# Own-place terms of two groups from scaled values, a one-step state update, and another order of work around the first bursts

## The reference

```python
for t in range(S):                      # attention with decay; state starts at 0
    y[:, :, t] = r_t . (state + (u * k_t) outer v_t)
    state = w * state + k_t outer v_t
x = y as 1536 rows of 384
p = probs / (sum(probs) + 1e-9)         # 4 experts
out = sum over e of p_e * (relu(x @ w1[e]) @ w2[e])     # 384 -> 1024 -> 384
h = out @ w_in;  result = (h * sigmoid(1.702 h)) @ w_out # 384 -> 2048 -> 384
```

## Time and profile before

| | us |
|---|---|
| median of 3 runs | 656.1 (653.75 to 657.89) |
| the profiled execution | 653.33 |
| its span, first to last instruction | 651.6 |
| PE busy in the span | 640.1 |
| DVE / ACT / POOL busy | 228.6 / 203.3 / 177.8 |
| mean granted clock of TensorE | 0.995 |

### The profile page before, as it was taken

The page is one execution under the profiler, slowest core; times in us unless marked ns, Lnnn a source line. Parts: engine busy times, 40 slices in busy tenths (PEclk is TensorE's granted clock), DMA queues, the critical chain, the costliest instruction groups (busy, mean ns, idle before and its releaser), DMA issues.

```text
span 651.6 us, 9471 instructions
## 1 busy us (share of the span) xinstructions
PE 640.1 (98%) x3886; PEld 540.4 (83%) x3887; DVE 228.6 (35%) x358; ACT 203.3 (31%) x429; POOL 177.8 (27%) x174
## 2 busy tenths in 40 slices
PE   7889999999999999999999999999999999999998
PEld 5789999988888888888888888888888888888886
DVE  8867666312122222222222222222543333333332
ACT  4544344232222211222211223222653333333332
POOL 6754320153234310434310436240770000000000
PEclk8999999999999999999999999999999999999999
DMA  8742343102300040100040000040000010001001
GB/s 312 297 154 86 128 175 133 52 2 94 149 1 1 12 184 0 49 0 1 9 185 1 0 1 1 11 185 0 1 0 1 1 48 1 1 1 48 1 1 48
DMA packets 8723, 38.69 MB, mean 59 GB/s; under 512 B 1504, under 2 KB 1632, under 8 KB 7392
## 3 DMA queue, kind: packets, MB, share of 16 engines
q1 hardware_dynamic: 8672, 38.00, 15.5%
HBM read 35.62 MB, written 2.38 MB: 58 GB/s over the span
## 4 chain that ended last, share of the span: by engine, by line
PE 95%; DVE 2%; issue 1%; ACT 1%; DMA 1%; SPq 0%; DVEq 0%; ACTq 0%
PE bank L1029 45%; PE bank L1053 30%; PE bank L1069 15%; PE bank L1099 2%; PE bank L1136 1%; PE bank L1139 1%; PE bank L1128 1%; ACT q_a_t L687 1%; DMA rk_in<-rk_t 1%; PE bank L1112 1%; DVE q_r_mid L760 0%; DVE q_a_t L842 0%; PE bank L1131 0%; DVE q_a_t L831 0%; DVE q_k_mid L757 0%
## 5 line engine op out<-in xcount | busy, mean ns | idle before, releaser
L1029 PE MATMUL bank<-x_hi,w_hi 128*128 128x512 f32 (+1 forms) x480 | 177.1, 369 | 0.2 <-DVE x_lo L779 0.2
L1029 PE MATMUL bank<-x_lo,w_hi 128*128 128x512 f32 (+1 forms) x480 | 177.0, 369 | 0.0
L1029 PE MATMUL bank<-x_hi,w_lo 128*128 128x512 f32 (+1 forms) x480 | 176.9, 369 | 0.0
L810 DVE SCALAR_TENSOR_TENSOR h_lo<-bank,h_hi 128x512 fp32r<-128x512 f32 (+1 forms) x112 | 68.8, 614 | 271.4 <-ACT h_hi L655 271.0
L655 ACT ACTIVATE h_hi<-bank 128x512 fp32r<-128x512 f32 (+1 forms) x112 | 59.9, 534 | 278.4 <-PE bank L1029 278.4
L579 POOL TENSOR_TENSOR w_lo<-staging,w_hi 128x384 fp32r<-128x384 f32 x80 | 82.2, 1039 | 167.5 <-ACT w_hi L625 167.5
L1053 PE MATMUL bank<-h_hi,w_hi 128*128 128x512 f32 (+1 forms) x336 | 121.9, 363 | 0.6 <-DVE h_lo L810 0.6
L1053 PE MATMUL bank<-h_lo,w_hi 128*128 128x512 f32 (+1 forms) x336 | 120.8, 360 | 0.0
L1053 PE MATMUL bank<-h_hi,w_lo 128*128 128x512 f32 (+1 forms) x336 | 120.8, 360 | 0.0
L1029 PEld LDWEIGHTS bank<-x_hi,w_hi 128*128 128x128 f32 x480 | 90.9, 189 | 15.3 <-issue 0.4
L1029 PEld LDWEIGHTS bank<-x_hi,w_lo 128*128 128x128 f32 x480 | 90.9, 189 | 14.9
(11 more groups left out here) (76 smaller groups left out, 447.5 us busy)
## 6 DMA issues: line engine op xcount, KB each, us to landing
staging<-weights SPq DMA_DIRECT2D x10, 1536.0 KB, 8.7
rk_in<-rk_t SPq DMA_DIRECT2D x12, 512.0 KB, 5.3
rkv_in<-rkv_n SPq DMA_DIRECT2D x10, 608.0 KB, 4.0
staging<-weights SPq DMA_DIRECT2D x4, 768.0 KB, 11.7
p_bc<-p_normalised SPq DMA_DIRECT2D x4, 768.0 KB, 4.4
out<-p_bc SPq DMA_DIRECT2D x9, 256.0 KB, 2.1
rkv_in<-rkv_n SPq DMA_DIRECT2D x2, 416.0 KB, 5.7
u_bc<-u_flat SPq DMA_DIRECT2D x1, 192.0 KB, 11.4
```

Of the source, the lines that this page charges most:

```text
L810: dve.scalar_tensor_tensor(h_lo[:, slot, 0:size], hid, 0.0, h_hi[:, slot, 0:size].bitcast(F32), ALU.max, ALU.subtract).then_inc(sem["hlo"], 1)
L1029: last = pe.matmul(bank[:, HID[j % 2], 0:tokens.stop - tokens.start], w[:, k, :], xs[c][:, k, tokens], start=(n == 0), stop=(n == 3 * KT - 1))
```

## The change

Groups 0 and 1 no longer have the own-place term in a_t. ACT zeroes `a_t[:, 0]` early, POOL zeroes `a_t[:, 1]`; DVE's `own_values` multiplies v by the result of first_diagonal, read from PSUM, into `v_first`, and PE adds it to the group's result with three 128x128 matmuls against the identity. ACT's `first_state` copies the first state. `carry` becomes four operations, one per pair of heads, new = old * w^128 + add; `fade` and `faded` go. The shares are made on DVE alone. Piece (f, 1) of the stage-0 weights gets its low part on DVE for f in 0, 1, 2, 7. v rows grow from 7 to 8 blocks of 16 per pair, u comes as 128 equal rows. The schedule is written out by hand up to group 5 and by a rule behind; the places and counts of bursts, hidden and output steps on PE stay as they are, but attend(2) now stands ahead of key_values(1), behind burst 1. SP issues rkv(2) and u ahead of the first half of w2, and the second half of w2 behind rkv(3).

The diff's core, its indentation reduced (`...` is left out; most of the removed lines stand in the functions above):

```diff
+LOW_BY_VECTOR = (0, 1, 2, 7)
...
 ALONE = 2
+SUMMED = 2
 JOIN = SMALLS * FT
-APART = 3
-BURST_AT = tuple(3 + APART * i for i in range(CH - ALONE))
+BURST_AT = tuple(3 + 3 * i for i in range(CH - ALONE))
+EARLY = ()
 Q = 32
-VW, SW = 7 * 16, 2 * D
+VW, SW = 4 * Q, 2 * D
 V_EVEN, V_ODD = slice(0, Q), slice(VW - Q, VW)
-V_REST = slice(Q, 2 * Q), slice(Q + 16, 2 * Q + 16)
+V_REST = slice(Q, 2 * Q), slice(2 * Q, 3 * Q)
 V_ALL = slice(0, D), slice(VW - D, VW)
...
+        v_first = [acc[:, c, PAIRS * P:PAIRS * P + DM] for c in range(SUMMED)]
...
+items = [("lead", 0), ("bonus", 1), ("values", 0), ("burst", 0), ("split", 0), ("products", 2), ("burst", 1),
+         ("split", 1), ("diagonal", 2), ("attend", 2), ("values", 1)]
+items.extend(("split", i) for i in range(2, FIRST))
+place = {}
...
+put(1, 0, ("fade", 2))
+put(1, 3, ("base", 2), ("scale", 3))
+put(1, 4, ("carry", 1), ("mask", 2), ("rest", 2))
+put(2, 2, ("products", 3), ("fade", 3))
+put(3, 2, ("diagonal", 3))
+put(3, 4, ("base", 3))
+put(4, 0, ("rest", 3), ("scale", 4))
+put(4, 1, ("carry", 2))
+put(4, 4, ("products", 4))
+put(5, 1, ("mask", 3))
+put(5, 2, ("fade", 4))
+put(5, 4, ("diagonal", 4), ("base", 4))
+put(6, 0, ("rest", 4))
+put(7, 1, ("mask", 4))
+put(7, 2, ("products", 5), ("carry", 3))
+put(8, 0, ("diagonal", 5))
+put(8, 1, ("fade", 5))
+put(8, 2, ("base", 5))
+put(8, 4, ("scale", 5))
+put(9, 2, ("carry", 4))
+put(11, 1, ("rest", 5))
+put(11, 4, ("mask", 5))
+put(13, 3, ("carry", 5))
+for c in range(6, CH):
+    a = BURST_AT[c - ALONE - 1]
+    put(a - 2, 1, ("products", c))
+    put(a - 1, 1, ("fade", c))
+    put(a - 1, 4, ("scale", c), ("diagonal", c))
+    put(a + 0, 2, ("base", c))
+    put(a + 1, 0, ("rest", c))
+    put(a + 2, 0, ("mask", c))
+    put(a + 4, 4, ("carry", c))
 for j in range(JOIN):
...
+    items.extend(place.get((j, 0), ()))
     items.append(("hidden", j))
...
+    items.extend(place.get((j, 1), ()))
     for part in STAGE0[FIRST:]:
         if part in ((j + 1, 1), (j + AHEAD, 0)):
             items.append(("split", STAGE0.index(part)))
...
+    items.extend(place.get((j, 2), ()))
+    if j in BURST_AT:
+        items.append(("burst", ALONE + BURST_AT.index(j)))
+    items.extend(place.get((j, 3), ()))
+    if j >= 1 and j - 1 not in EARLY:
         items.append(("output", j - 1))
...
+    if j in EARLY:
+        items.append(("output", j))
+    items.extend(place.get((j, 4), ()))
...
 load_half(0, 0)
+load_rkv(2)
+sp.dma_start(u_bc[:, :], u_rows).then_inc(sem["urow"], 16)
 load_half(0, 1)
-load_rkv(2)
-sp.dma_start(u_bc[:, :], u_flat.to_broadcast([P, DM])).then_inc(sem["urow"], 16)
 load_half(1, 0)
...
     for c in range(CH - XBUF):
         sp.wait_ge(keys_sem(c), keys_count(c))
-        if c < ALONE:
+        if c < SUMMED:
             sp.wait_ge(sem["q_rk"], c + 1)
         load_rk(c + XBUF)
+        sp.wait_ge(sem["q_w"], c + 1)
+        if c == 1:
+            sp.wait_ge(sem["q_kv"], 2)
+        load_rkv(c + XBUF)
         if c == 0:
             load_half(1, 1)
-        sp.wait_ge(sem["q_w"], c + 1)
-        load_rkv(c + XBUF)
         if c == 2:
             store_probs()
             sp.wait_ge(sem["pdone"], 16)
...
+    pool.memset(a_t[:, 1], 0.0).then_inc(sem["q_clear"], 1)
+    def first_fade(c):
         pool.wait_ge(s_rkv[c], 16)
         fade_keys(c).then_inc(sem["q_kn"], 1)
...
+    pool.wait_ge(sem["q_rk"], ALONE)
+    first_fade(0)
+    first_fade(1)
+    first_keys()
     for what, i in SCHEDULE:
...
+        if what == "products" and i < CH:
+            products(i, "q_ru", "q_ruk", SUMMED)
+        elif what == "fade" and i < CPB * 2 - 1 and i % CPB < CPB - 1:
+            fade_keys(i).then_inc(sem["q_kn"], 1)
+        elif what == "split" and STAGE0[i][1] and STAGE0[i][0] not in LOW_BY_VECTOR:
             rest_low(i)
...
+act.activation(a_t[:, 0].rearrange("p g x t -> p (g x t)"), zeros[:, :].to_broadcast([P, 2 * PAIRS * P]),
+               ACT.Copy).then_inc(sem["q_zero"], 1)
...
+        act.wait_ge(sem["q_diag"], c + 1 - SUMMED)
+        act.wait_ge(sem["q_w"], c - 1)
         for p in range(PAIRS):
             last = act.activation(a_t[:, c % 2, g, p, :], ident[:, :], ACT.Identity,
                                   scale=ruk_sb[:, c % 2, 2 * p + g:2 * p + g + 1])
         last.then_inc(sem["q_base"], 1)
...
+    def first_state():
+        act.wait_ge(sem["q_kv"], 1)
+        act.activation(state[:, 1], bank[:, KV_BANK, 0:PAIRS * SW].rearrange("p (x d) -> p x d", x=PAIRS),
+                       ACT.Copy).then_inc(sem["q_st"], 1)
+    first_state()
     for what, i in SCHEDULE:
         if what == "burst":
             x_high(i, "q_w", i + 1, y_bank(i))
-        elif what in ("ready", "base") and i < CH:
+        elif what == "base" and i < CH:
...
+def shares():
+    dve.tensor_reduce(psum_sb[:, 0, :], probs_sb.rearrange("p e j -> p j e"), mybir.AxisListType.X, ALU.add).then_inc(sem["psum"], 1)
...
+    def own_values(c):
+        dve.wait_ge(s_rkv[c], 16)
+        dve.wait_ge(sem["q_d"], c + 1)
+        own = d_of(c).rearrange("p (x g) -> p x g", x=PAIRS).unsqueeze(3)
+        halves, parts = (v_in[:, c].rearrange("p x (n d) -> p x n d", d=d) for d in (Q, D - Q))
+        dve.tensor_tensor(v_first[c][:, 0:H * Q].rearrange("p (x g d) -> p x g d", x=PAIRS, g=2),
+                          halves[:, :, 0::3], own.to_broadcast([P, PAIRS, 2, Q]), ALU.mult)
+        dve.tensor_tensor(v_first[c][:, H * Q:].rearrange("p (x g d) -> p x g d", x=PAIRS, g=2),
+                          parts[:, :, 2:6:3], own.to_broadcast([P, PAIRS, 2, D - Q]), ALU.mult).then_inc(sem["q_vd"], 1)
     def causal(c, g):
         dve.wait_ge(sem["q_a"], c + 1)
...
+        if c == 0:
+            dve.wait_ge(sem["q_zero"], 1)
+        elif c == 1:
+            dve.wait_ge(sem["q_clear"], 1)
+        elif c < SUMMED:
+            dve.wait_ge(sem["q_w"], c - 1)
         else:
-            dve.wait_ge(sem["q_base"], 2 * c + g - 1)
+            dve.wait_ge(sem["q_base"], 2 * (c - SUMMED) + g + 1)
         dve.copy_predicated(a_t[:, c % 2, g], after[:, :].bitcast(U32).unsqueeze(1).to_broadcast([P, PAIRS, P]),
                             bank[:, a_banks(c)[g], :].rearrange("p (x t) -> p x t", x=PAIRS)).then_inc(sem["q_tri"], 1)
     def carry(c):
         ci = c % CPB
-        new, add = state[:, (ci + 1) % 2], bank[:, KV_BANK, 0:PAIRS * SW].rearrange("p (x d) -> p x d", x=PAIRS)
+        old, new = state[:, ci % 2], state[:, (ci + 1) % 2]
+        add = bank[:, KV_BANK, 0:PAIRS * SW].rearrange("p (x d) -> p x d", x=PAIRS)
         dve.wait_ge(sem["q_kv"], states(c))
         if ci == 0:
             dve.tensor_copy(new, add).then_inc(sem["q_st"], 1)
         else:
-            dve.wait_ge(sem["q_fade"], states(c - 1))
-            dve.tensor_tensor(new, faded[:, :, :], add, ALU.add).then_inc(sem["q_st"], 1)
-    def fade(c):
-        dve.wait_ge(sem["q_st"], states(c))
-        dve.tensor_tensor(faded[:, :, :], state[:, (c % CPB + 1) % 2], w_pow[:, :, P:P + 1].to_broadcast([P, PAIRS, SW]),
-                          ALU.mult).then_inc(sem["q_fade"], 1)
+            dve.wait_ge(sem["q_st"], states(c - 1))
+            for p in range(PAIRS):
+                last = dve.scalar_tensor_tensor(new[:, p], old[:, p], w_pow[:, p, P:P + 1], add[:, p], ALU.mult, ALU.add)
+            last.then_inc(sem["q_st"], 1)
     def diagonal_of(c):
...
+        if c >= SUMMED + 2:
+            dve.wait_ge(sem["q_base"], 2 * (c - SUMMED - 1))
+        diagonal(c, "q_ruk", "q_diag", SUMMED)
...
     key_products(0)
     scale(1)
     key_products(1)
-    own_base(0)
+    causal(0, 0)
     causal(0, 1)
-    causal(0, 0)
-    own_base(1)
-    carry(0)
+    own_values(0)
+    causal(1, 0)
     causal(1, 1)
-    causal(1, 0)
+    own_values(1)
+    shares()
     for what, i in SCHEDULE:
         if what == "burst":
-            if i >= ALONE and i % CPB < CPB - 1:
-                carry(i)
             x_low(i, y_bank(i))
...
+        elif what == "diagonal" and i < CH:
             diagonal_of(i)
-            if i == 2:
-                carry(1)
-        elif what == "scale":
+        elif what == "carry" and i % CPB < CPB - 1:
+            carry(i)
+        elif what == "scale" and i < CH:
             scale(i)
-            fade(1)
         elif what == "mask" and i < CH:
             causal(i, 0)
             causal(i, 1)
...
+        elif what == "split" and (STAGE0[i][1] == 0 or STAGE0[i][0] in LOW_BY_VECTOR):
...
-                last = pe.matmul(y_rest(y_bank(c), p), v_in[:, x, p, V_REST[g]], a_t[:, c % 2, g, p, :], start=False, stop=(g == 1))
+                last = pe.matmul(y_rest(y_bank(c), p), v_in[:, x, p, V_REST[g]], a_t[:, c % 2, g, p, :], start=False,
+                                 stop=(g == 1 and c >= SUMMED))
+        if c < SUMMED:
+            pe.wait_ge(sem["q_vd"], c + 1)
+            for k in range(KT):
+                last = pe.matmul(bank[:, y_bank(c), k * P:(k + 1) * P], v_first[c][:, k * P:(k + 1) * P], ident[:, :],
```

(17 more changed lines are left out.)

182 lines of the change are left out of this document (44 added, 138 removed).

## The result

The changed kernel took 645.92 us (median of 4 executions, 645.87 to 646.00); the kernel before, run beside it, 654.92 us (4, 652.63 to 657.89). The profiled execution took 645.87 us with a span of 643.9.

What follows compares the result with a forecast made beforehand. DVE's order of work in the first bursts was taken as the limit. Head 0.5 + 6.03 - 0.4 left at burst 2 = 6.1 us, off the median 656.1: 650.0 us forecast, range 646.5 to 655.0.

Steps and rivals of the forecast that it cites:

- What bounds the kernel: Whole run: PE busy 98% of the span; from 18 to 125 us, DVE's order of work in the first bursts is the limit.
- The 6.03 us between 21 and 55 us: First output to end of attend 5: 6.03 us lost, 2.13 by attend 3's end and 3.90 in the next period.
- The state in four operations: carry(1) in burst 2: four 96-column operations take 0.95 us; DVE gains 0.4 us per group, of no use to later groups.
- own_values: Head, on DVE: two operations of 256 and 128 columns, 0.7 us each, bounds 0.5 and 1.4, done before PE asks.
- The head: Start up to the first output: gain 0.5 us, bounds -0.4 and +1.0, with added matmuls at 0.45 + 0.3 us.
- The sum, carried to the median: Whole kernel: gain 6.1 us makes the profiled 653.33 us 647.2; the same gain off the median 656.1 gives 650.0.
- Rival C: Head: half-clock stretch at 11 us ends earlier or H0 follows attend(2) at once; gain 7.5 us, 648.6; chance 0.09.
- Rival A: Clock still falls once, elsewhere, perhaps from small matmuls and waits in bursts 1 and 2; price 1.5 us, 651.5; chance 0.16.
- B: Burst 2 or 3: DVE or ACT is late, 1 to 1.5 us each; gain 3 us, 653; chance 0.15.
- D: Nine later bursts: ACT's base and rest around x_high delay the next step and PE; 7.4 us slower, 663.5; chance 0.03.
- E: The change does nothing: waits only move to the state (carry) and h_lo in front of it; 656; chance 0.05.

## Why the prediction was wrong

The direction held, and so did the place and the mechanism of the larger part, the waits behind the first output. The size did not: 650.0 forecast, 645.9 measured, 4.1 us off and below a range that began at 646.5. Two steps failed: the term of the head, which took the half-clock stretch at 11 us as standing and priced the added matmuls too low, and the step from the profiled execution to the median. By the prediction's own steps:

- **What bounds the kernel.** Right. DVE was late for the waits of the earlier trace rows, PE's work made the rest: with the waits gone PE is busy 106.96 of 107 us.
- **The 6.03 us between 21 and 55 us.** Right, and a little more: 6.25 us went. The working left 0.4 us at burst 2 (0.3 for the state, 0.1 for the masks). None was left: scale(3), taken as 1.36 us, was done by 22.8 where the working had 24.3, the state by 23.7 (25.25) and the masks by 24.96 (26.6); and the steady period is 9.92 instead of 10.01, twice.
- **The state in four operations.** 0.98 us against 0.95. The Trainium skill's page "VectorE: DVE Perf Modes", section on the TRN2 errata, gives an estimated 1.03 by its fixed part per instruction, from a formula that it states for a tensor_tensor addition; the row lies between the two, and the 0.1 us that it stood for does not show. The gain of 0.4 us per group on DVE was said to be worth nothing later; undone in the new order it costs 0.4 us in all at full clock.
- **own_values.** 0.40 + 0.27 us from start to end, as taken (0.7), with POOL busy beside it. The rule of the Trainium skill's page "SBUF — State Buffer", section "SBUF: two separate sides", said so: the exclusive lock on the port shared with POOL is for DVE operations with two SBUF inputs, and these have one in PSUM. The trace agrees, and own_base, when put back for group 1 alone, took 1.68 us beside POOL.
- **The head** was the first wrong step: a gain of 0.5 us, "bounds -0.4 and +1.0", and it gave 1.5. Two terms were off in opposite directions. The three matmuls a group take 0.86 us, 1.72 in all, not 0.75: I had priced them by attend's run, 16 in 1.16 us, whose matmuls have 48 rows. And the half-clock stretch at 11 us was taken as standing ("the first three fall in the half-clock stretch that stands there now"). It wasn't there in the profiled execution; where it is, in the second profile of this kernel, the matmuls take 1.58 and 0.87 us, the first output starts at 20.99, and nothing of the 0.5 us is left (21.02 before). That this execution took 647.41 us, next to the 647.2 of the working, is luck: the head's missing 0.5 us makes up for what burst 2 and later gave beyond the sum.
- **The sum, carried to the median,** was the larger error. The working gave an own time of 647.2 for the profiled execution, and 645.87 came: 1.3 us off, the head's 1.0 and the 0.6 of the stretch behind it, less 0.25 us outside the span. To this I added the 2.8 us by which the median of before, 656.1, lies over its profiled execution, 653.33, as if "the same gain" applied. But 656.1 is the median of three executions, and that of 79 is 653.8. By the clocks, the spread is half-clock stretches that come and go between executions, and those behind bursts 2 and 3 went with the waits. Before ran from 652.3 to 658.1 us over the 79 executions, the changed kernel from 645.7 to 647.5 over 10. From 653.8 the same working would have given 647.7, an estimate, 1.8 us off instead of 4.1.

Of the 9.0 us between the medians (654.92 and 645.92), 651.2 - 645.9 = 5.3 us are waits and work, by the estimate at full clock, and about 4 us the clock. Rival C, "The head gives more", had the right mechanism ("the half-clock stretch at 11 us ends earlier") and the right gain for one execution, 7.5 us, and 0.09 of the chance; it too was carried over to 656.1, which put it at 648.6. Rival A (the clock still falls once) happens in 2 of 10 executions, in the head, for its price of 1.5 us. What was held against it, that the clock stayed up behind the waits at 40 to 44 us, did not hold in the second profile of before. B, D and E did not come. (In D, 9 x 0.7 is 6.3, not 6.1; nothing else hangs on it.)

What stays open: why, with the same instructions in the same order, the head has the half-clock stretch in some executions and not in others. It goes with the pace of the transposes at 5 us or the wait at 6, but no kernel here moved either by itself; and with the old order of loads all six executions have the clock that goes with it. How much of the gain is the new order by itself is open too, since no run has it alone, and the split of the 9 us into waits and clock is an estimate by a line through the executions of before.

## What to carry to other kernels

When the time of a kernel before varies by 1% between executions and the trace shows half-clock stretches of TensorE, work out what part of the spread the change removes, before you add a gain to a median: the gain belongs to the clock level of the execution it was worked out from. On a kernel whose bound engine is 98% busy, look for the waits of 1 to 2 us in its first stretch and for the order of the engine that makes them; their removal was worth more than their length here (PE idle for 6.7 us less, the span 7.7 us shorter, with 1.7 us of matmuls added). When you put a wait or a stretch down to an edit, look where it lies: a median can be worse by a stretch that comes ahead of the place of the edit. And undo the parts one at a time before you call one of them the cause: here own place alone did nothing in the kernel before, and was worth 1.5 us in the changed one.
